# Removing the 64- and 128-byte offsets from the on-chip buffers of the expert stage (attention and two mixtures, one core)

## The reference

```python
q_s = softmax(q, axis=-1); k_s = softmax(k, axis=seq)
x = q_s @ (k_s^T @ v)                      # per batch and head, then heads side by side: 2304 x 512
a = x @ w1; b = x @ w2                     # 512 -> 1024
x = ((a * b) @ w3) @ w_out                 # 1024 -> 1024 -> 512
p = domain_probs / (domain_probs.sum(-1) + 1e-9)
out = sum over 4 experts e of p[:, e] * (relu(x @ W1[e]) @ W2[e])   # 512 -> 1024 -> 512
```

## The kernel before

| buffer | role | before | after |
|---|---|---|---|
| `w12` high, low | stationary, second stage | 0, 0 | 0, 0 |
| `xy` high, low | moving | the same for both, multiples of 512 | same |
| `w3t`, `wout` high, low | first stage | 0, 0 | 0, 0 |
| `uf` | stationary, expert stage | 64 | 0 |
| `tx[0]`, `tx[1]` | moving | 0, 2048 | 0, 2048 |
| `tx[2]` | moving | 128 | 0 |
| `hT` | stationary | 0 | 0 |
| `u2` high, low | moving | 2176, 2304 | 1408, 1408 |
| `sums` | GpSimd scratch | 2304 | 1408 |
| `snap` | running sums | 2304 | 1408 |
| `pg` | output factors | 1408 | 1920 |

## Time and profile before

### The profile page before, as it was taken

How to read it: one execution, slowest core, us unless ns; L and a number is a source line. 1 busy time by engine, 2 the same in 40 slices (tenths; PEclk the granted TensorE clock), 3 DMA queues, 4 the chain that set the end, 5 groups by cost and what they waited for, 6 DMA issues and landing times.

```text
span 1200.3 us, 15947 instructions
## 1 busy us (share of the span) xinstructions
PE 1165.8 (97%) x6112; PEld 1069.7 (89%) x6112; DVE 611.3 (51%) x900; ACT 295.5 (25%) x565; POOL 298.2 (25%) x358
## 2 busy tenths in 40 slices
PE   7788899999999989999999999999999999999998
PEld 6677899999999988899999998998999999999997
DVE  5988432121221385555555555555555555555555
ACT  4436531121111232222221211212222222212111
POOL 2334710000000311422322422323223223224210
PEclk9889999999999989999999999999999999999999
DMA  9686320000000100100100001001001001010012
GB/s 269 140 166 136 88 64 1 1 0 0 0 0 0 35 0 1 36 19 17 35 3 32 29 7 35 17 17 35 17 17 35 17 18 35 2 33 27 9 53 105
DMA packets 45453, 46.56 MB, mean 39 GB/s; under 512 B 22640, under 2 KB 36976, under 8 KB 45424
## 3 DMA queue, kind: packets, MB, share of 16 engines
q1 hardware_dynamic: 45424, 46.18, 14.2%
HBM read 41.46 MB, written 4.72 MB: 38 GB/s over the span
## 4 chain that ended last, share of the span: by engine, by line
PE 89%; DVE 5%; DMA 2%; ACT 2%; issue 1%; SPq 0%; DVEq 0%
PE b_ring L1070 9%; PE b_ring L1072 8%; PE b_ring L1071 8%; PE b_w L1070 7%; PE b_w L1072 7%; PE b_w L1071 7%; PE b_kv L1070 5%; PE b_kv L1072 5%; PE b_kv L1071 5%; PE b_w3t L1070 4%; PE b_kmax L1070 4%; PE b_kmax L1071 4%; PE b_kmax L1072 4%; PE b_w3t L1072 4%; PE b_w3t L1071 4%; DMA kb<-in_k 2%
## 5 line engine op out<-in xcount | busy, mean ns | idle before, releaser
L1031 DVE SCALAR_TENSOR_TENSOR acc<-b_ring,pg,acc 128x512 f32<-128x512 f32 x180 | 135.1, 751 | 111.1 <-PE b_ring L1072 111.1
L412 POOL TENSOR_SCALAR uf<-stage 128x256 fp32r<-128x256 f32 x48 | 19.6, 407 | 566.2 <-PE b_kmax L1072 232.7
L1070 PE MATMUL b_ring<-u_hi,hT 128*128 128x512 f32 x384 | 150.9, 393 | 0.0
L1072 PE MATMUL b_ring<-u_hi,hT 128*128 128x512 f32 x384 | 150.2, 391 | 0.0
L1071 PE MATMUL b_ring<-u_lo,hT 128*128 128x512 f32 x384 | 149.1, 388 | 0.0
L615 ACT ACTIVATE hT<-b_w 128x384 fp32r<-128x384 f32 x72 | 35.4, 492 | 451.1 <-DVE b_w L1009 446.9
L1031 DVE SCALAR_TENSOR_TENSOR acc<-b_kv,pg,acc 128x512 f32<-128x512 f32 x90 | 67.6, 751 | 60.8 <-PE b_kv L1072 60.7
L1072 PEld LDWEIGHTS b_ring<-u_hi,hT 128*128 128x128 f32 x384 | 71.8, 187 | 16.8
L1071 PEld LDWEIGHTS b_ring<-u_lo,hT 128*128 128x128 f32 x384 | 72.1, 188 | 15.8
L1070 PEld LDWEIGHTS b_ring<-u_hi,hT 128*128 128x128 f32 x384 | 72.2, 188 | 15.0
L1070 PE MATMUL b_kv<-u_hi,hT 128*128 128x512 f32 x192 | 75.7, 394 | 0.2 <-issue 0.2
(11 more groups left out here) (170 smaller groups left out, 2774.6 us busy)
## 6 DMA issues: line engine op xcount, KB each, us to landing
stage<-in_moe_w SPq DMA_DIRECT2D x40, 512.0 KB, 3.3
qb<-in_q SPq DMA_DIRECT2D x4, 1152.0 KB, 9.4
kb<-in_k SPq DMA_DIRECT2D x4, 1152.0 KB, 9.3
vb<-in_v SPq DMA_DIRECT2D x32, 144.0 KB, 3.9
out<-acc SPq DMA_DIRECT2D x18, 256.0 KB, 2.0
stage<-in_moe_w SPq DMA_DIRECT2D x16, 256.0 KB, 3.2
wraw<-in_moe_w_out SPq DMA_DIRECT2D x4, 512.0 KB, 6.6
pr<-in_moe_domain_probs SPq DMA_DIRECT2D x1, 36.0 KB, 4.2
```

Source lines behind the costliest of these rows:

```text
L412: nc.gpsimd.tensor_scalar(uf[:, form, HI], of, 1.0, 0.0, ALU.mult, ALU.add).then_inc(pool_hi, 1)
L1031: nc.vector.scalar_tensor_tensor(acc[:, tile, :], O_BANK[t % TT], scale, acc[:, tile, :], ALU.mult, ALU.add).then_inc(acc_added, 1)
L1070: nc.tensor.matmul(ps, w_hi_, x_hi_, start=start, stop=False, skip_group_check=onto)
L1072: return nc.tensor.matmul(ps, w_lo_, x_hi_, start=False, stop=stop, skip_group_check=onto)
```

## The change

Addresses alone change. No instruction, wait, loop or transfer is added, taken away or moved; the two tensors `u2_hi` and `u2_lo` become one tensor with the high part first.

```diff
-    TX_AT = [AT + 40960, AT + 59392, AT + 16384 + 128]
+    TX_AT = [AT + 40960, AT + 59392, AT + 16384]
...
-    uf = at("uf", [P, 7, 2, 2, P], F32R, AT + 64)
+    uf = at("uf", [P, 7, 2, 2, P], F32R, AT)
...
-    pg = at("pg", [P, NT, NG // 2], F32, EX)
-    U2 = EX + 768
-    u2 = [at("u2_hi", [P, 2, DM], F32R, U2), at("u2_lo", [P, 2, DM], F32R, U2 + 4224)]
-    sums = at("sums", [P, 4, 2, P], F32, U2 + 8320)
-    snap = at("snap", [P, 3, TB], F32, U2 + 12416)
-    b11_last = at("b11_last", [P, 2, TB], F32, U2 + 12416)
+    u2 = at("u2", [P, 2, 2, DM], F32R, EX)
+    sums = at("sums", [P, 4, 2, P], F32, EX + 8192)
+    snap = at("snap", [P, 3, TB], F32, EX + 12288)
+    b11_last = at("b11_last", [P, 2, TB], F32, EX + 12288)
+    pg = at("pg", [P, NT, NG // 2], F32, EX + 16896)
...
-                nc.gpsimd.tensor_scalar(u2[HI][:].rearrange("p c n -> p (c n)"), stage[:, 1, :], 1.0, 0.0,
+                nc.gpsimd.tensor_scalar(u2[:, HI].rearrange("p c n -> p (c n)"), stage[:, 1, :], 1.0, 0.0,
                                         ALU.mult, ALU.add).then_inc(pool_u2, 1)
                 pool.wait_ge(pool_u2, g + 1)
-                nc.gpsimd.tensor_tensor(u2[LO][:].rearrange("p c n -> p (c n)"), stage[:, 1, :],
-                                        u2[HI][:].rearrange("p c n -> p (c n)").bitcast(F32),
+                nc.gpsimd.tensor_tensor(u2[:, LO].rearrange("p c n -> p (c n)"), stage[:, 1, :],
+                                        u2[:, HI].rearrange("p c n -> p (c n)").bitcast(F32),
                                         ALU.subtract).then_inc(u2_ready, 1)
...
-                                     u2[HI][:, j, :], u2[LO][:, j, :], j == 0, j == 1)
+                                     u2[:, HI, j, :], u2[:, LO, j, :], j == 0, j == 1)
```

## The result

The changed kernel takes 1212.47 us in the median of 7 runs (1208.45 to 1214.18), the kernel before 1202.94 us in 7 (1202.06 to 1205.63). The ratio is 1.0061, with a 95% interval from 1.0047 to 1.0076: slower by 0.6%, 7.3 us by the ratio. The medians of these seven and seven are 9.5 us apart; the changed kernel was executed ten more times, and the median of all 17 is 1210.72 us. The forecast was 1203.2 us and no measurable change; the time lies above the range.

The account below looks back on a forecast made before the run. PE was taken as the bound, 97% busy and almost without waits in the expert stage. Terms of 0 and +0.3 us for the products, against the 1202.94 us median, gave 1203.2 us, no measurable change; range 1199.5 to 1209.8 us.

Parts of the forecast that it names:

- the second rival: GpSimd's split of `u2` needs over 0.38 us longer, PE waits 15 times; 3.3 us at 0.60 us longer; chance 0.03.
- The term of `sums`, `snap` and `pg`: VectorE and ScalarE accesses to these moved buffers: slack covers small changes, up to 0.6 us an operation; 0.
- the term of `u2`: Moving operand of 1728 `project` matmuls of 512 columns: distance between starts unchanged at 229.1 ns, so 0; upper bound 5.9 us.
- the comparison: First two stages as models of the new layout: aligned buffers there show 229.1 and 173.3 ns, no different from now.
- the mean: First stage, 23 matmuls from 25.22 to 30.26 us: 22 distances in 5.04 us, taken as 229.1 ns each.
- a faster case of 5.3 us: Rival of a measurable gain, 4.3 us of it in `project`, 2.5 ns for each matmul; chance 0.09.
- slower, by the streams of PE: Rival: with all buffers aligned, products keep 176.7 ns; 6.9 us more, 12.8 with `project` too; chance 0.17.
- its 5.9 us for `project`: Share of the PE-streams rival in `project`: 1728 matmuls at 3.4 ns more each.
- The term of the products: Expert-stage products reading `uf` and `tx[2]`: six more matmuls of 3.4 ns in each of 16 groups; +0.3 us.
- the prediction's reading that 0 and 64 make no difference for `uf`: Products at 173.3 ns in the second stage (shift 0) and the expert stage (`uf` shifted 64), so no visible difference.

Follow-up runs that it names:

- `hT` up 128: Changed kernel with both parts of the stationary `hT` moved to places 128 bytes up and `tx[2]` making room at 14336; 1200.81 us, ratio 0.9978.
- both parts up 128: Changed kernel with high and low `u2`, and `sums`, `snap`, `pg`, moved up 128 bytes, parts still 4096 apart; 1201.83 us, ratio 0.9974.
- two best layouts: The runs `hT` up 128 and both parts up 128, each made on the changed kernel; 1200.81 and 1201.83 us.
- the low part alone: Kernel before with only the low part of `u2` moved, to 4096 bytes behind the high part instead of 4224; 1214.19 us, ratio 1.0089.
- half of the blocks at 0: Changed kernel with 128 bytes also between the halves of each `u2` part, so four blocks lie 2176 bytes apart; 1209.46 us, ratio 1.0041.

## Why the prediction was wrong

The views that said what bounds the kernel were read rightly: PE without waits, so that only the distance between matmuls or a new wait could move the time. There was no new wait, and the split of `u2` on GpSimd kept its time (min/median/max in ns), against 2390/2406/2406 in the earlier trace rows:

```profile
L421 POOL TENSOR_TENSOR u<-stage,u x16: 2392/2392/2402, 408.5 to 1158.8; 128x1024 fp32r<-128x1024 f32 x16
```

So the second rival, a slower split, was not what happened. The term of `sums`, `snap` and `pg` was right at 0: with `hT` up 128 they lie just as in the changed kernel, and the time is 1200.81 us, 0.9978 of the kernel before.

The step that failed is the term of `u2`, "The term is 229.1 less 229.1, so 0". Measured, it is 233.3 less 229.1, some 7 us. The step had two faults.

The first is the comparison. The prediction says: "The layout that the change makes is the one that the other two stages have today". For `w12`, `xy`, `w3t` and `wout` that means aligned against each other, stationary against moving. For `u2` it meant only high against low. The change puts `u2` at 1408 bytes past a multiple of 4096 and leaves `hT` at 0. 1408 is 5 x 256 + 128, so both parts of the moving operand lie 128 bytes off the stationary one, which they do in none of the pairs just named. The table of offsets ahead of the prediction had the numbers; I compared the wrong pair. In the kernel before, the low part at 2304 = 9 x 256 was the only one aligned to `hT`, and the change took this away. Two runs bear it out from both sides: give the 128 bytes back to `u2` or to `hT`, and `project` takes 8.20 and 8.19 us.

The second is the mean. The 22 distances of the earlier trace rows average 229.1 ns, the same as `project`, and I took this for one pace. The rows in between show two:

```profile
25.22 0.40 PE L1071 MATMUL b_w<-wout_lo,w3t_hi 128*128 128x512 f32 x1
...
27.31 0.39 PE L1071 MATMUL b_w<-wout_lo,w3t_hi 128*128 128x512 f32 x1
...
30.26 0.39 PE L1072 MATMUL b_w<-wout_hi,w3t_lo 128*128 128x512 f32 x1
```

Nine distances to 27.31 us take 2.09 us, 232 ns each. The last 13 take 2.95 us, 226.9 ns each. This aligned stream runs at 226.9 ns once it has settled, and that of the run with both parts up 128 at 226.7. Had I split this stretch, I would have seen that `project` at 229.1 was not at the pace of an aligned stream and that its layout already cost something. The two best layouts take a part of that cost away in `project` (8.25 to 8.20 and 8.19 us), which gives 0.2 to 0.3% (0.9974 and 0.9978). The lower end of the range, 1199.5 us, is reckoned from a faster case of 5.3 us, 4.3 of it for `project`, 2.5 ns for each matmul. No run shows what this 2.5 ns was worked out from; what the two best layouts showed in its place is 47 `project`s that take 2.2 and 2.7 us less in sum, 1.3 to 1.6 ns for each matmul.

Of the rival nearest to what happened, "slower, by the streams of PE", the direction was right and the mechanism the wrong way round. It held that buffers at aligned addresses would be slow, in the products first, and had a chance of 0.17. In the runs it is misalignment that is slow (8.39 to 8.40 us at differences of 128 or 192, 8.19 and 8.20 at 0), and the loss lies in `project`. That its 5.9 us for `project` came near the 7.0 measured is luck: its 3.4 ns for each matmul were read from the products.

The term of the products, +0.3 us, was wrong too; measured, it is -0.6 us. It rests on the stretch with 7.34 us, which the prediction took for the only slow one and laid to GpSimd or to the buffer that is read. Two stretches, the first of the kernel before and the second of the run with the low part alone, speak against GpSimd (its busy time is the 6.33 and the 1.14 us):

```profile
777.61:784.89 7.28, 7.28 (x43) 7.28 (x42) 4.13 (x7) 2.52 (x6) 6.33 (x6) 1.00 0.23 72
705.00:712.40 7.40, 7.40 (x43) 7.40 (x42) 4.12 (x7) 2.52 (x6) 1.14 (x2) 1.00 0.00 1
```

With GpSimd busy for most of the stretch the products can be fast, and with GpSimd almost idle they can be slow. What the slow stretches share is `uf` at 64. With it the same products have two paces, 173.3 and 176 to 177 ns. The last row shows this as well, and the prediction did not use it: that stretch runs on to 738.25 us, 7.45 us in all. A distance of 0.28 us after the start at 734.98 us interrupts the stream (such a gap, of 0.23 to 0.28 us, comes in about every second group, in both kernels), and the product at 736.14 us takes 1.06 us (first two lines). In the changed kernel the gap is the 0.23 us after 737.69 us, and the like product takes 1.04 us (last two):

```profile
736.14 0.34 PE L1070 MATMUL b_kmax<-xy_hi,uf 128*128 128x384 f32 x1
737.20 0.34 PE L1070 MATMUL b_w<-tx,uf 128*128 128x384 f32 x1
738.81 0.33 PE L1069 MATMUL b_kmax<-xy_hi,uf 128*128 128x384 f32 x1
739.85 0.33 PE L1069 MATMUL b_w<-tx,uf 128*128 128x384 f32 x1
```

So the prediction's reading that 0 and 64 make no difference for `uf` held only for the fast pace. With `uf` and `tx[2]` alone at 0 the 7.34 us went away (735.5 against 736.2 us for the stage). Behind a slow `project`, `uf` at 64 gives 7.33 to 7.40 us in most stretches (low part alone) and `uf` at 0 gives 7.29 us (the changed kernel). Which of `uf` and `tx[2]` matters in the 7.34 us, where the slow pace begins with the product on `tx[2]` at 717.29 us, was not separated.

**What stays open.** Why the difference between the moving and the stationary operand matters was not shown; the runs show that it does: with no other engine's work changed, 128 bytes on the stationary or on the moving side move `project` from 8.19 to 8.39 us and from 8.20 to 8.40 us. The period of 256 bytes rests on a shift of 768 bytes that changed nothing (8.25 us, a ratio of 1.0004) and on two good layouts (8.20 and 8.19 us) whose differences, 1536 and 1280 bytes, are both multiples of 256, while 128 and 192 are bad (8.39 to 8.40 us). For `project` a difference of 64 was not tried, and neither was `hT` at 128 with `u2` at 0: that the difference counts, and not some fast places of `hT` and `u2` each, rests on three of the four combinations, and on the products, which are slow (7.39 us in place of 7.29) with `uf` at 128 and what they read at 0. How mixed differences add up is not explained: half of the blocks at 0 gave 8.36 us, one part in two at 0 gave 8.24. The two kinds of matmul also depend on each other. In the run with the low part alone the products take 7.40 us with nothing of theirs moved, and `project` takes 8.36 us where the changed kernel has 8.40 at the same differences; in the two fastest runs the products take 7.31 us in place of 7.29. How one stream passes this on to the next is open.

## What to carry to other kernels

Where PE is the bound and never waits, compare the distance between starts with that of the best settled stretch of the same shape, not with a mean. If it is above, look at the offsets of the stationary and the moving operand modulo 256 bytes and make them equal before anything else is tried; here it was worth 0.8% between two kernels that differ by 128 bytes in the place of `hT` alone (1.0059 and 0.9978 of the kernel before). Such a change can be worth little: against the kernel before, the two best layouts gain 0.2 to 0.3%. And a buffer is aligned only against a named other one: high against low said nothing here (4096 bytes apart both at 8.20 and at 8.40 us for `project`), stationary against moving nearly all (8.19 or 8.20 against 8.40).

## What the runs showed of the hardware that was not expected

Matmuls of 512 columns with new weights for each start some 227 ns apart at a granted clock of 1.00 when both operands agree modulo 256 bytes, after the first five (`hT` up 128: 230, then 227.1 ns) or nine (`u2` up 128: 231, then 226.7 ns). They start 233.3 ns apart when the operands differ by 128 or 192 (8.39 to 8.40 us for 36), with longer and shorter distances in turn (0.24, 0.23, 0.24 and 0.22 us in the changed kernel). Matmuls of 384 columns go from 173.6 to 176.0 ns when `uf` is 128 bytes off (42 of them in 7.29 and 7.39 us). With `uf` 64 bytes off, 42 of them take 7.28 us in one stretch and 7.34 or 7.40 in another, without any wait; with `uf` at 0 the stretch that took 7.34 takes 7.29.
